# Weights of two feed-forward networks: split in place from large unsplit loads instead of through stage buffers

## What is computed

```
# 1 gated recurrent attention (computed in blocks of 128 tokens)
m_new = max(f_t + m, i_t);  f' = exp(f_t + m - m_new);  i' = exp(i_t - m_new)
C = f' * C + i' * outer(v_t, k_t);   n = f' * n + i' * k_t
y_t = sigmoid(o_t) * (C @ q_t) / max(|n . q_t|, 1)
# 2 rational feed-forward, w_in 320x2048, w_out 2048x320
h = x @ w_in;  P = a0 + a1*h + a2*h^2 + a3*h^3
g = P / (1 + |b0|*|h| + |b1|*h^2 + 1e-6);   x = g @ w_out
# 3 normalised and gated, w_gate and w_val 320x1536, w_out 1536x320
xn = x / rms(x) * rms_g;  u = xn @ w_gate
out = (u * sigmoid(u) * (xn @ w_val)) @ w_out
```

## Time and profile before

| | |
|---|---|
| median of 3 runs | 536.94 us (535.34 to 537.94) |
| profiled execution, its own time | 538.72 us |
| its span | 536.9 us |
| mean granted TensorE clock | 0.927 |
| busy: TensorE | 495.3 us (92%) |
| busy: VectorE | 328.2 us (61%) |
| busy: ScalarE | 302.0 us (56%) |
| busy: GpSimd | 232.5 us (43%) |
| read from HBM | 24.37 MB |

### The profile page before, as it was taken

One profiled execution on the slowest core, in us unless ns is written; L12 is line 12 of the kernel. 1 busy time (PEld: TensorE's weight loads), 2 busy tenths in 40 slices (PEclk: granted clock), 3 DMA queues, 4 the chain that ended last, 5 costly groups with the idle time before them and its releaser, 6 DMA issues.

```text
span 536.9 us, 7362 instructions
## 1 busy us (share of the span) xinstructions
PE 495.3 (92%) x2646; PEld 434.7 (81%) x2646; DVE 328.2 (61%) x467; ACT 302.0 (56%) x500; POOL 232.5 (43%) x260
## 2 busy tenths in 40 slices
PE   3997987988769999999999988999999999999996
PEld 2796876878548989889978977888888888888886
DVE  8435545455488999998998974545544434443343
ACT  8484664561488999899986966683422122221211
POOL 3033545353337998678874674848810000000000
PEclk9999557667788999999998999999999999999999
DMA  7913334551000010000000010423201000010001
GB/s 206 312 33 116 114 114 122 165 171 32 0 0 1 1 29 15 1 2 1 0 1 1 1 31 12 127 83 85 66 1 50 0 1 0 1 49 2 0 1 49
DMA packets 13168, 26.81 MB, mean 50 GB/s; under 512 B 1740, under 2 KB 8012, under 8 KB 13132
## 3 DMA queue, kind: packets, MB, share of 16 engines
q1 hardware_dynamic: 13132, 26.34, 16.5%
HBM read 24.37 MB, written 1.97 MB: 49 GB/s over the span
## 4 chain that ended last, share of the span: by engine, by line
PE 69%; issue 7%; DVE 6%; POOL 5%; ACT 4%; DMA 1%; DVEq 0%; POOLq 0%; ACTq 0%
PE ps L1267 6%; PE ps L1268 6%; PE ps L1266 6%; PE ps L1209 5%; PE ps L1211 5%; PE ps L1210 5%; PE ps L1192 4%; PE ps L1229 4%; PE ps L1228 4%; PE ps L1227 4%; PE ps L1194 4%; PE ps L1193 4%; PE ps L1270 3%; PE ps L1271 3%; PE ps L1195 2%
## 5 line engine op out<-in xcount | busy, mean ns | idle before, releaser
L779 ACT ACTIVATE ab<-ps 128x512 f32<-128x512 f32 x36 | 21.6, 599 | 112.5 <-PE ps L1271 112.4
L504 POOL TENSOR_TENSOR qq<-qq,ab 128x512 f32<-128x512 f32 x48 | 61.2, 1296 | 52.6 <-ACT qq L706 52.6
L1036 DVE TENSOR_TENSOR ab<-ps,ab 128x512 f32<-128x512 f32 x36 | 24.9, 691 | 86.0 <-ACT ab L779 86.0
L511 POOL TENSOR_TENSOR g_lo<-cc,g_hi 128x512 fp32r<-128x512 f32 x48 | 61.4, 1302 | 8.7 <-ACT g_hi L727 8.7
L1209 PE MATMUL ps<-wo_hi,g_hi 128*128 128x320 f32 x192 | 59.9, 312 | 5.5 <-POOL g_lo L511 3.7
L1211 PE MATMUL ps<-wo_hi,g_lo 128*128 128x320 f32 x192 | 59.6, 311 | 0.0
L1210 PE MATMUL ps<-wo_lo,g_hi 128*128 128x320 f32 x192 | 59.6, 311 | 0.0
L1192 PE MATMUL ps<-x_hi,w_hi 128*128 128x512 f32 x96 | 40.7, 424 | 8.2 <-DVE cc L971 8.1
L1229 PE MATMUL ps<-wo_hi,g_lo 128*128 128x320 f32 x144 | 44.5, 309 | 0.0
L1228 PE MATMUL ps<-wo_lo,g_hi 128*128 128x320 f32 x144 | 44.5, 309 | 0.0
L1227 PE MATMUL ps<-wo_hi,g_hi 128*128 128x320 f32 x144 | 44.4, 308 | 0.0
(11 more groups left out here) (187 smaller groups left out, 1303.8 us busy)
## 6 DMA issues: line engine op xcount, KB each, us to landing
stage<-w_in_dram SPq DMA_DIRECT2D x15, 384.0 KB, 4.3
qk<-q_k_dram SPq DMA_DIRECT2D x12, 416.0 KB
stage<-w_out_dram SPq DMA_DIRECT2D x8, 320.0 KB, 3.1
kn<-k_n_dram SPq DMA_DIRECT2D x12, 208.0 KB, 4.6
v<-v_n_dram SPq DMA_DIRECT2D x12, 164.0 KB, 4.8
sig_o<-o_n_dram SPq DMA_DIRECT2D x2, 960.0 KB, 11.4
qq<-w_in_dram SPq DMA_DIRECT2D x5, 384.0 KB, 3.2
out_dram<-y_out SPq DMA_DIRECT2D x12, 160.0 KB, 1.9
```

The source lines that it names most:

```text
L504: pool.tensor_tensor(qq[m % 2][:, h, :], qq[m % 2][:, h, :], ab[m % 2][:, h, :], ALU.mult)\
L511: pool.tensor_tensor(glo(n), cc[m % CR][:, n % 2, :], ghi(n).bitcast(F32), ALU.subtract)\
```

## The change

The stage buffers are gone. The low part of a weight has the size of the unsplit weight, so the unsplit weight is loaded straight into the home of its low part (`w1_raw` is the same memory as `w1_lo`, `wo1_raw` as `wo1_lo`, and so on: `in_place`). ScalarE rounds from there into the high part, and the subtraction reads and writes the low part's home in place. Only the twice-held rows have a buffer of their own (`rest1_raw`, later `rest2_a` in the same place, and `rest2_b`). Loads take four tiles (input: 512 KB, output: 640 KB; the rest rows of eight tiles: 512 KB). None of the first network's loads waits for a semaphore; they stand between the attention loads in SyncE's queue. The host lays the input weights out as a main and a rest array.

Rounding starts one block later on ScalarE (it = 2) and the splits at it = 3; the rest rows are rounded and split for four tiles at a time, in every second period. The second half of the output gates is taken at it = 5. The stage homes being gone, `FA` is 4 (`w2b` has 2 tiles, `w2c` 6), and all four tiles of `w2a` are split early: 12 steps in turns 3 to 14 of GpSimd's loop. The late loads wait for `h_done` 48 (output weights, `w2b`) and `out_done` 48 (`w2c`, one load of 1.5 MB). Four constants for the start move from the home of `wo1` to that of `x_hi`, since `wo1` is now loaded early.

```diff
-EARLY = 2
-        stage = [at(f"stage{i}", [P, 6 * P]) for i in range(2)]
+        rest_at = cursor[0]
+        rest1_raw = at("rest1_raw", [P, FT1, P])
+        rest2_a = at("rest2_a", [P, FT1 // 2, 2 * P], F32, offset=rest_at)
+        def in_place(name, shape):
+            offset = cursor[0]
+            return at(name + "_lo", shape, F32R), at(name + "_raw", shape, F32, offset=offset)
...
-        w1_lo = at("w1_lo", [P, FT1, 2 * P], F32R)
+        w1_lo, w1_raw = in_place("w1", [P, FT1, 2 * P])
-        wo1_lo = at("wo1_lo", [P, FT1, HD], F32R)
+        wo1_lo, wo1_raw = in_place("wo1", [P, FT1, HD])
...
-            def load_piece(n):
-                kind, f, m = pieces[n]
-                if 2 <= n < LATE + 2:
-                    wait_split(sp, n - 2)
-                elif n >= LATE + 4:
-                    wait_split(sp, n - 4)
-                elif n >= 2:
-                    sp.wait_ge(qr_done, NP + n - LATE - 3)
-                src = {"in1": w1_in, "out1": w1_out, "out2": w2_out, "in2": w2_in}[kind][:, f:f + m, :]
-                sp.dma_start(staged(n, src.shape[2]), src).then_inc(stage_in[stage_slot(n)], 16)
+            def load_main1(g):
+                part = slice(4 * g, 4 * g + 4)
+                sp.dma_start(w1_raw[:, part, :], w1_main[:, part, :]).then_inc(main1_in[g], 16)
+            def load_rest1(g):
+                part = slice(8 * g, 8 * g + 8)
+                sp.dma_start(rest1_raw[:, part, :], w1_rest[:, part, :]).then_inc(rest1_in[g], 16)
+            def load_out1(g):
+                part = slice(4 * g, 4 * g + 4)
+                sp.dma_start(wo1_raw[:, part, :], w1_out[:, part, :]).then_inc(out1_in[g], 16)
...
+            sp.wait_ge(rest1_ready, 4)
+            sp.dma_start(rest2_a[:, :, :], w2_rest[:, 0:FT1 // 2, :]).then_inc(rest2_in[0], 16)
+            sp.wait_ge(xlo_done, NT)
+            sp.dma_start(w2_a[3][:, :, :], w2_main[:, 0:FA, :]).then_inc(main2_in[0], 16)
+            sp.dma_start(rest2_b[:, :, :], w2_rest[:, FT1 // 2:, :]).then_inc(rest2_in[1], 16)
+            sp.wait_ge(h_done, NB * FT1)
+            for g in range(3):
+                part = slice(4 * g, 4 * g + 4)
+                sp.dma_start(wo2_raw[:, part, :], w2_out[:, part, :]).then_inc(out2_in[g], 16)
+                if g == 0:
+                    sp.dma_start(w2_b[3][:, :, :], w2_main[:, FA:FA + FB, :]).then_inc(main2_in[1], 16)
+            sp.wait_ge(out_done, NB * FT1)
+            sp.dma_start(w2_c[3][:, :, :], w2_main[:, FA + FB:, :]).then_inc(main2_in[2], 16)
...
+            def split_main1(p):
+                part = slice(2 * p, 2 * p + 2)
+                pool.wait_ge(main1_hi, p + 1)
+                pool.tensor_tensor(w1_lo[:, part, :], w1_raw[:, part, :], w1_hi[:, part, :].bitcast(F32), ALU.subtract)\
+                    .then_inc(main1_ready, 1)
...
-                if 3 <= k < 3 + 3 * EARLY:
+                if 3 <= k < 3 + 3 * FA:
                     split_early(*divmod(k - 3, 3))
...
-                if it == 4:
+                if it == 5:
                     output_gates(1)
                 if it >= 2:
                     hi_of_x(it - 2)
-                for _ in range(2):
-                    if it >= 1 and piece < NP1:
-                        round_piece(piece)
-                        piece += 1
+                if 2 <= it < 2 + PB:
+                    round_main1(it - 2)
+                    if it % 2 == 0:
+                        round_rest1((it - 2) // 2)
+                    round_out1(it - 2)
```

More of the change, by code:

```diff
@@ L285, in build @@
         y2_sent = [sem(f"y2_sent{i}") for i in range(TT)]
[L288 to L318, removed]
-            return 16 * ((n - LATE) // 4 + 1 + (LATE // 2 if stage_slot(n) < 2 else 0))
-        def staged(n, width):
-            slot = stage_slot(n)
-            home = stage[slot][:, :] if slot < 2 else qq[slot - 2][:, :, :].rearrange("p a n -> p (a n)")
-            m = pieces[n][2]
-            return home[:, 0:m * width].rearrange("p (f n) -> p f n", f=m)
         def w2(f):
@@ L330, in w2, with w2_part, rest2 @@
             return w2_b + (f - FA,) if f < FA + FB else w2_c + (f - FA - FB,)
+        def w2_part(f):
+            return 0 if f < FA else 1 if f < FA + FB else 2
+        def rest2(f):
+            return rest2_a[:, f, :] if f < FT1 // 2 else rest2_b[:, f - FT1 // 2, :]
+        late = []
+        for f in range(FT2):
+            late.append(("out2", f))
+            if f >= 1 and FA + f - 1 < FT2:
+                late.append(("in2", FA + f - 1))
         block = ctx.enter_context(nc.Block())
@@ L552, in _ @@
                     rms(slice(0, TT), 1)
-                if 3 <= k < 3 + 3 * EARLY:
+                if 3 <= k < 3 + 3 * FA:
                     split_early(*divmod(k - 3, 3))
             pool.wait_ge(glo_done, NB * FT1)
-            for n in range(LATE, len(pieces)):
-                split(n)
-                if n == LATE + 9:
+            for n, (kind, f) in enumerate(late):
+                split_late(kind, f)
+                if n == 9:
                     rms(slice(TT, NT), 2)
-                if LATE + 9 <= n < LATE + 9 + TT:
-                    gains(TT + n - LATE - 9)
+                if 9 <= n < 9 + TT:
+                    gains(TT + n - 9)
             for t in range(2 * TT, NT):
@@ L665, in _ @@
             weights(0)
-            piece = 0
             for it in range(NT):
@@ L769, in _ @@
                     rms_start(slice(0, TT), TT)
-            round_piece(LATE)
-            round_piece(LATE + 1)
+            round_late(*late[0])
+            round_late(*late[1])
             def sigmoid(n):
@@ L795, in _ @@
                 for _ in range(2):
-                    if piece < len(pieces):
-                        round_piece(piece)
+                    if piece < len(late):
+                        round_late(*late[piece])
                         piece += 1
```

207 lines of the change are left out of this document (118 added, 89 removed).

## The result

The changed kernel took **504.36 us** (median of 4 executions, 504.02 to 513.54), the kernel before 537.44 us beside it (535.34 to 542.28): a ratio of 0.937, 95% interval 0.929 to 0.945. Ratios here leave out executions over 1.5% above the fastest of their kernel, such as the one of 513.54 us. The profiled execution took 504.02 us with a span of 502.2 us; its granted clock was 0.989 on average. Forecast were 515 us and a range of 503 to 531; what came is the time of rival A, 506 us.

The account below looks back on a forecast made before the run. The prediction took weight loads waiting for splits to bound the attention loop, largely through TensorE's clock. Loop -20.1 and tail -1.5, the rest 0, sum to -21.6 us: 517.1 against the profiled execution, 515 us against the median, range 503 to 531.

Parts of the forecast that it names:

- rival A: Attention loop: the clock stays up after the sigmoid, giving 506 us; chance 0.22.
- my main step: Attention loop: without TensorE's waits, such as 2.28 us for the exponential, the clock's falls go; nearly all the gain.
- the ring: Attention loop: exponential, VectorE's work, its split, DMA of about 3 us, rounding, next exponential; some 10 us a period.
- the period with the sigmoid: Loop period with two table loads on ScalarE: 10.0 us, TensorE waiting some 3 us for x_lo, and the clock falls.
- two periods at the lower level: Loop behind the sigmoid: clock low until it rises, 22.2 us for two periods of 11.1.
- tail of attention: End of attention, 123.2 to 133.8 us: 1.9 us shorter at the upper clock level, taken as -1.5.
- C: Attention loop: TensorE becomes the bound at its lower clock level, 11.1 us a period; +9 us, 546 us; chance 0.05.
- step 2: SyncE's queue: 960 KB more weights ahead of block 4's rows, 3.1 us; taken as 0, ends 0 and +3.1.
- step 3: GpSimd in the first feed-forward: four early tiles split instead of two; taken as 0, ends 0 and +1.0.
- step 4: Late weights: two fewer tiles split late, tiles 6 to 11 loaded after the first network's last product; taken as 0.
- B: Attention loop: new waits of TensorE, 1 to 2 us a period, keep the clock near half and half; 523 us; chance 0.24.
- D: Attention loop: the wait only changes its name, larger loads coming too late; 533 to 538 us; chance 0.04.

Follow-up runs that it names:

- two-tile loads: Changed kernel with first-network loads cut to two tiles each, a pair behind each block's rows, without waits for the splits: 506.32 us, ratio 0.937 to the kernel before.
- two early tiles: Changed kernel with two tiles of the second network split early instead of four, the others late: 507.01 us.
- gates once: Changed kernel with both halves of the output gates taken through the sigmoid at block 1, so no table loads stand in the loop: 508.97 us.
- gates once and x_lo first: Changed kernel with output gates taken in one go at block 1, x_hi ahead of spreading and x_lo ahead of the state update: 507.53 us.
- x_lo first: Changed kernel with x_hi ahead of the spreading of gates on ScalarE and x_lo ahead of the state update on VectorE: 506.10 us.
- 12 copies in block 7: First try at delaying an exponential: changed kernel with 12 repeated copies of x_hi on ScalarE in block 7: 509.10 and 518.25 us.
- 5 copies in block 3: Changed kernel with 5 repeated copies of x_hi on ScalarE in block 3, holding up the next exponential: 507.89 us.
- three stage buffers: Kernel before with three stage buffers instead of two, so a load waits for the split of the third piece back: 510.08 us, ratio 0.945.
- 12 copies in block 3: Changed kernel with 12 repeated copies of x_hi on ScalarE in block 3, holding up the next exponential: 518.55 us.
- 9 copies in block 3: Changed kernel with 9 repeated copies of x_hi on ScalarE in block 3, holding up the next exponential: 514.45 us.

## Why the prediction was right, and where it was not

**The bound was read rightly.** SyncE's waits for the splits set the period: put back by themselves they give back the time of before, a little more in fact (541.19 against 537.96 us), and taken away by themselves they give the whole gain (506.32 us). That bare waits were the smaller part of it and the clock the larger also held: 8.6 against 24.9 us. Of my main step, "take such waits away and such falls go", the loop as a whole bears out the direction (0.67 of the clock with the ring, 0.80 and more without). As a statement on single waits and single falls it doesn't hold: a wait of 3.30 us passed without a fall, and a fall came with no wait over 0.6 us in the 20 us ahead. The ring was drawn through the weights alone, though. The attention rows stood behind the same waits, GpSimd waited 37.7 us for them, and no run took one of the two waits away without the other. For the gain it makes no difference, as the change removes both.

**Luck had a part in the range.** The forecast of 515 us, with 0.45 the likeliest case, did not come; 504.4 us is near rival A, which had 0.22. It lies even below A's 506, and the low end of 503 does not follow from the parts, since all their open costs could only add time. Only the 0.5% between runs, 2.7 us, carries the range there.

**The sum, term by term** (forecast, measured in the profiled execution):

| part | forecast | measured |
|---|---|---|
| three periods at the upper level | 20.1 | 18.3 (37.35 to 55.61) |
| the period with the sigmoid | 10.0 | 9.5 (to 65.08) |
| two periods at the lower level | 22.2 | 11.1 (to 76.20) |
| two at the upper level | 13.4 | 13.4 (to 89.65) |
| the eight periods | 65.7 (-20.1) | 52.3 (-33.5) |
| tail of attention | -1.5 | +0.3 |
| the rest, steps 2 to 4 | 0 | -1.5 |
| in all | -21.6 | -34.7 |

**The step that failed** is "two periods at the lower level until it rises". In the profiled execution TensorE waited 1.52 us for x_lo behind the sigmoid, not the "some 3 us" that I put there, and the clock stayed up until 98.6 us. These 11.1 us are nearly the whole miss. The forecast case does exist: in the kernels with two-tile loads and with two early tiles TensorE waited 1.53 us in the same place, and the clock fell at 65.7 for 10.2 us. Even so the exponentials then came at 65.70, 74.83 and 81.36 us (two early tiles), 15.7 us for two periods and not 22.2, and the first network's product at 105.5, 5 us later than in the changed kernel. So the term was too large there even where its condition held. In the first kernel with 12 copies, the same program as the changed kernel up to that place, the clock fell after 1.53 us where the changed kernel's stayed up after 1.52: whether the term comes at all is not settled by the length of that wait, and what settles it stays open. The changed kernel's slowest execution, 513.54 us, would fit such a fall, but no trace of it exists, and others with as low a mean clock took 505 us.

The size was taken from the kernel before, with its low spells of 6.9 and 27.1 us, as "one to two and a half periods". Without the ring the loops' first spells were 6.8 to 23.9 us, and 20.5 us (gates once) and 23.9 us (gates once and x_lo first) came with no wait over 1.3 us in the 20 us ahead. With the gates once, two periods in a low spell took 21.9 us (63.54 to 85.47), the size of the term. The size is therefore within what comes, and no run shows that the program decided that the profiled execution had none.

**The smaller misses.** The period at the upper level came from one period of before with 0.32 us of waiting in it, 6.65; measured are 5.6 to 6.2 us for five of the seven plain ones and 6.8 and 6.6 for the last two. The tail didn't gain: the clock fell in it, at 98.6, so 1.9 us of it were low (3.8 before), and TensorE's waits for x_lo in it grew from 1.57 to 2.65 us. The 1.5 us gained behind attention belong to no part of my working, and no run here settles from what they come. C's sum takes the tail as 3.4 us longer, which is not what its own numbers give: counted by the two shares, 1.00 and 0.50, "never high" makes the 6.8 us at the upper level twice as long, 6.8 and not 3.4 us more. Measured is 14.6 us instead of 10.6 in the execution at the lower level, so the 3.4 were nearer, by luck.

**The costs at nothing.** SyncE's order (step 2): no engine waits for a load of attention rows in the loop, and two-tile loads give no other time. GpSimd's early splits (step 3): about 0.5 us at most, by the run with two tiles. The late weights (step 4): inside 401.7 us against 403.1.

**The rivals.** A was the outcome in time. The sigmoid's wait was shorter than thought, as it argued (1.52 us), but that this kept the clock up is not shown, since it fell after 1.53 us elsewhere. Nor do the traces show that a busy TensorE brings the upper level back, or when: it was busy 20.50 us of 20.50 at 0.50 with the moved gates, and 887.0 of 906.1 us in the execution that never left the lower level. B is out: TensorE's waits for x_lo sum to 6.1 us in the whole run, none over 1.6, and the loop's clock was 1.00. D is out: no copy waits for a DMA. C's price of the loop was right, 11.43 us a period where I had 11.1 and 91.4 us for the loop, the very end that I had given it. But it came once in ten executions of the changed kernel, with a clock that was low in the networks too (907.88 us and not 546), and nothing shows that the missing waits had to do with it.

## What to carry to other kernels

Where TensorE waits a few times per loop, look at the granted clock before you add up the waits: here 8.6 us less of idle time in TensorE went with 24.9 us less of matmul time. Do not read a fall of the clock as the price of one wait, however: falls came after waits of 0.9 to 4.1 us, and once with none over 0.6 us in the 20 us ahead, while waits of 3.3 us passed without one. When loads and splits share two buffers, follow the ring once around (split, load, rounding, next work), and see what else stands in the same queue behind the load that waits. Here one more buffer broke it (510.08 us) as well as loads straight into their home (504.36), and loads of two tiles did as well as those of four (506.32 against 504.36). Once the loop's clock is up, a single fall can cost more than the next few microseconds of removed work (the eight periods took 57.2 us with a low spell of 10.2 us in them, 52.3 with none): judge such edits by what the engines do in the trace, and by many executions.

## What the runs showed of the hardware

- The program alone did not fix where the granted clock fell. These are the first falls from 36 us on in the kernels without the ring, one profile each: where the clock went from 1.00 to 0.50, for how long, how long TensorE was busy in that spell, and its last wait of over 0.2 us ahead, with the time from its end to the fall:

| kernel | fell at, us | low for, us | TensorE busy, us | last wait ahead, us |
|---|---|---|---|---|
| the change | 98.6 | 6.8 | 6.80 of 6.80 | 1.56, ended 1.1 ahead |
| two-tile loads | 65.7 | 10.2 | 10.10 of 10.10 | 1.53, 0.3 |
| two early tiles | 65.7 | 10.2 | 10.20 of 10.20 | 1.53, 0.3 |
| x_lo first | 65.6 | 6.8 | 6.80 of 6.80 | 0.88, 1.8 |
| gates once | 66.8 | 20.5 | 20.50 of 20.50 | 1.27, 1.2 |
| 12 copies in block 7 | 67.8 | 17.1 | 17.10 of 17.10 | 1.53, 3.0 |
| 5 copies in block 3 | 68.6 | 6.8 | 6.80 of 6.80 | 2.30, 2.6 |
| gates once and x_lo first | 85.4 | 23.9 | 23.09 of 23.80 | 0.52, 3.0 |
| three stage buffers | 55.8 | 23.9 | 22.46 of 23.90 | fell in a wait of 3.25 (to 57.24) |
| 12 copies in block 3 | 52.3 | 10.2 | 10.20 of 10.20 | 4.07, 0.4 |
| 9 copies in block 3 | 60.3 | 6.8 | 6.90 of 6.90 | 1.97, 2.2 |

  The kernels with copies in block 7 and with two early tiles have exactly the changed kernel's instructions ahead of their falls at 67.8 and 65.7, where the changed kernel's clock stayed at 1.00 up to 98.6. Nor did the length of the last wait go with that of the spell: 6.8 us came behind 0.88 and behind 2.30 us, 10.2 behind 1.53 and behind 4.07.
- The rise moved as well. In the changed kernel's profile it came at 37.2 us, with 9 copies at 50.1, and the period before it took 11.09 us (exponentials at 37.62 and 48.71); with 12 copies in block 3 and with three stage buffers the clock was up from 25.0 to 28.4 us already, and again from 35.3.
- One execution of the changed kernel passed wholly at the lower level, by the lengths of its matmuls: 907.88 us. Its profile holds no record of the clock and prints 1.00 for it, while the mean of line 1246's matmuls was 501 instead of 314 ns.
- Ahead of the first entry of the clock's record, 1.00 is printed as well. In the changed kernel's profile that entry is at 37.2 us, and the 16 score matmuls of a block show the lower level before it:

```profile
28.43 2.08 PE L1138 MATMUL ps<-qk 40*128 40x128 f32 x16
...
38.42 1.16 PE L1138 MATMUL ps<-qk 40*128 40x128 f32 x16
```

  So the 1.00 of 13.40 to 26.80 us in the earlier trace rows, and in every mean clock given here the share of the time ahead of that first entry (25.0 us in two profiles, 50.1 with 9 copies, 37.1 to 39.5 in the others that have a record), are no reading of the clock.
- VectorE's split of an output piece, always of the same form, took 0.81 to 2.12 us in the changed kernel (minimum, median and maximum in ns, then first and last start):

```profile
L969 DVE TENSOR_TENSOR wo_lo<-wo_raw,wo_hi x8: 814/998/2119, 50.1 to 97.3; 128x640 fp32r<-128x640 f32 x8
```

No engine waited for its result. The two longest (2.12 us at 77.49 and 1.96 at 84.13) lie in the two periods that took 6.8 and 6.6 us, where VectorE goes on to the next block only behind them. That they made those periods longer, and what stretches them, was not tried.
